# A soft-capped attention and a squared-ReLU feed-forward on one core: another order of the seven products, and sums' transfers on ScalarE's queue

## The chip, the cores and the metric

One core of a Trainium2 chip. The metric is the device time of one launch in microseconds: the median of the runs shown. The profile is one further execution under the hardware profiler; its engines are TensorE (PE; its weight loads PEld), VectorE (DVE), ScalarE (ACT), GpSimd (POOL) and SyncE (SP), which only issues DMAs.

## The reference

For 4 batches, 12 heads, 448 positions and head size 64, everything in fp32:

```
scores = tanh(q k^T / 8 / cap) * cap
attn   = softmax(scores) v                    # per head
x      = heads side by side: 1792 x 768
h      = relu(x w_in)                         # w_in 768 x 2048
g      = s * h^2 + b
y      = g w_out                              # w_out 2048 x 768
```

## The kernel before

**Numbers.** fp32 precision is reached with pairs of fp32r values: every operand of the two big layers is split into a high part (rounded) and a low part (the rest), and a product is three matmuls: hi*hi, lo*hi, hi*lo. ScalarE mostly makes the high parts, DVE the low ones.

**Attention and layer 1.** The 24 pairs of heads are worked off one after another, and beside the attention of a batch TensorE works on layer 1 of the batch before: 16 hidden tiles (128 features x 448 positions), each of 6 x 3 matmuls (L715 to L717), two PSUM banks in turn. ScalarE takes the ReLU out of PSUM (`rectify`, L907) and squares it (L910) into one of three buffers, and SyncE stores it to `hidden_scratch` (`store_hidden`). Behind the last pair of heads the 16 hidden tiles of batch 3 remain: a stretch of TensorE work with little beside it.

**Layer 2** is a fast matrix product of the Strassen-Winograd kind. y is cut in halves of its features (3 accumulators of 128 each), the contraction over 2048 in two halves (8 tiles each), and the positions in batches; a pair of batches (0,1) or (2,3) gives one 2 x 2 problem, solved with seven products instead of eight. A step is one product i (0 to 6) for one pair (0 or 1): 8 tiles of g, each used in 3 x 3 matmuls (L741 to L743, 9 starts). 14 steps are 112 tiles and 1008 matmuls. The order is product by product, each for pair 0 and then pair 1. Tiles are numbered n from 0 to 111 throughout.

The products 3 to 6 need sums of hidden tiles, and 2 to 5 sums of weight tiles. GpSimd makes them in one buffer, `work`: two loads, four adds or subtracts (L1247 to L1253, or L1238 to L1244 for weights), two stores to `t_scratch` or `s_scratch`, and only then the next item. 24 items are listed in `COMBINED`: eight of weights, eight of each pair. SyncE issues their loads (`combine_load`, L388) and stores (`combine_store`, L409); a load waits until the item before has landed in DRAM, a store until GpSimd is done.

**The pipeline of a g tile n.** SyncE loads the raw tile into one of 7 buffers (`load_g`) once ScalarE and DVE are done with tile n-7. ScalarE makes x_hi = s*raw + b (`g_high`, L925; L927 where the product needs no b) in a ring of 6 tiles, once TensorE is done with tile n-6. DVE makes x_lo: for biased products (i < 4) s*raw + b first (L1097), then minus x_hi (L1102); for others one instruction (L1105). Weights come in steps of two tiles: a load (`load_w_out`), w_hi on ScalarE (L915), w_lo on DVE (L1089), 28 steps in all. They go into the place of w_in as its tiles are used up, four products' worth.

**Where products end.** Each step's three accumulators are taken out of PSUM: products 0 and 2 by a copy on ScalarE (`copy_out`), the others by sums on DVE (`add_up`, L1115 to L1139). y is put together in 18 tiles that lie where attention's buffers were (`y_places`), and SyncE stores them (`store_y`). Each pair has three banks of its own; a step waits for the step of its pair before.

**Who does what when** is written out by hand, in each engine's own program. SyncE, in the last stretch of layer 1: three weight steps and g tiles 0 to 6 first; then, for each of 16 hidden tiles, its store, at places a further weight step, and at every fourth a store and a load of a sum. In layer 2 it runs over n: a g load, at places a weight step, a store of y, and every eighth tile a store and a load of a sum, all in one queue. ScalarE and DVE convert four weight steps and g tiles 0 to 5 beside layer 1, the rest in layer 2.

Of the kernel before, what the change touches and what calls it, by code (L numbers as in the profile page):

```python
# [61 lines left out]
STEPS = PRODUCTS * HALVES  # L62
LAST = STEPS * HALF

BIASED = 4 * HALVES * HALF
# [8 lines left out]
COMBINED = ([(-1, k) for k in range(6)] + [(0, k) for k in range(HALF)] + [(-1, k) for k in range(6, HALF)]  # L74
            + [(1, k) for k in range(HALF)])
# [4 lines left out]
def attention_ffn(nc, lead, q_k, v, w_in, w_out, y_t):  # L80
# [5 lines left out]
    with ctx:  # L86
# [56 lines left out]
        y_places += [turned[:], xt[:], r_sum[:, 0, :], r_sum[:, 1, :], e_sum[:, 1, 0, :], e_sum[:, 1, 1, :]]  # L143
        y_places += [hidden_sb[:, u, :] for u in range(3)] + [v_flat[:, u * S:(u + 1) * S] for u in range(2)]
# [64 lines left out]
        p_copied = sem("p_copied")  # L209
# [53 lines left out]

        def hidden_tile(n):
            return hidden_sb[:, n % 3, :]
# [17 lines left out]
        def acc(pair, d):  # L283
            return (scores[:, d, :] if pair == 0 else scores[:, ACCS, :] if d == 0 else pv[:, d - 1, :])[:, 0:S]
# [34 lines left out]
        def free_w_place(eng, m):  # L319

            i, t = divmod(m, W_STEPS)
            if i < W_BUFFERS:
                eng.wait_ge(hid_done, (B - 1) * JT + W_STEPS * i + t + 1)
            else:
                eng.wait_ge(out_used, HALVES * HALF * (i - W_BUFFERS + 1))
# [7 lines left out]
        def w_step_at(n):  # L333

            m, off = divmod(n - RING, W_STEPS)
            m += W_STEPS
            return m if off == 0 and m < W_STEPS * PRODUCTS else None

        def step_at(n):

            step, off = divmod(n - RING + 1, HALF)
            return step - 1 if off == 0 and step > 0 else None

# [3 lines left out]
        def _(sp):  # L347
# [36 lines left out]
            def store_hidden(n):  # L384
                sp.wait_ge(sq_done, n + 1)
                sp.dma_start(hidden[n % JT, :, n // JT * S:(n // JT + 1) * S], hidden_tile(n)).then_inc(hidden_out[n % 3], 16)

            def combine_load(m):  # L388
                pair, k = COMBINED[m]
                if m == 0:  # L390

                    sp.wait_ge(w_in_lo, PIECES)
                else:
                    sp.wait_ge(combine_out, 32 * m)
                if pair >= 0:
                    for batch in (2 * pair, 2 * pair + 1):
                        for j in (k, HALF + k):
                            n = batch * JT + j
                            sp.wait_ge(hidden_out[n % 3], 16 * (n // 3 + 1))
# [582 lines left out]
        def _(dve):  # L982
# [208 lines left out]
            for m in range(W_STEPS):  # L1191
                w_out_low(m)
# [91 lines left out]
```

## Time and profile before

| | us |
|---|---|
| median of 3 runs (lowest, highest) | 599.15 (598.55, 599.56) |
| the profiled execution's own time | 600.41 |
| its span, first to last instruction | 598.6 |
| TensorE with a matmul under way | 587.4 (98%) |
| DVE | 428.2 (72%) |
| ScalarE | 338.3 (57%) |
| GpSimd | 180.1 (30%) |

The profiled execution has 1.8 us outside its span. A share over the whole span hides the stages: the windows below show some of them. Matmuls overlap, so a matmul of some 365 ns starts each 203 ns, and the starts, not the durations, show the pace. The granted clock is 1.00 nearly throughout.

### The profile page before, as it was taken

To read this page: it belongs to the slowest core of one execution; us is meant where nothing else is said; L and a number is where in the kernel's file an instruction comes from. 1 tells how busy PE (TensorE), PEld (TensorE's weight loads), DVE (VectorE), ACT (ScalarE), POOL (GpSimd) and SP (SyncE) were. 2 spreads that over 40 slices of the span, in tenths; PEclk is the share of its full clock that TensorE was granted. 3 is DMA by queue.
4 is the path that set the end of the run, shared out by engine and by line. 5 is a ranking of instruction groups with operands and counts; after the bars stand their busy time and mean duration, and the time that the engine had idled before them with its cause. 6 is when DMAs were issued, how large, how long until landed. Compare 5 with 4: busy or idle time off the path is not lost.

```text
span 598.6 us, 8830 instructions
## 1 busy us (share of the span) xinstructions
PE 587.4 (98%) x3074; PEld 467.9 (78%) x3074; DVE 428.2 (72%) x645; ACT 338.3 (57%) x406; POOL 180.1 (30%) x143
## 2 busy tenths in 40 slices
PE   8999999999999999999999999989999999999997
PEld 4335768677877868868769999979988998999996
DVE  5986999977686869778872033359999889766652
ACT  7985775775575575575652344455545554444430
POOL 0114976303433343434343332333333330000000
PEclk9999999999999999999999999999999999999999
DMA  8432454443545455565445967498898887766532
GB/s 295 154 111 71 120 166 158 133 149 138 191 175 212 163 193 211 208 211 213 165 150 192 350 219 230 178 332 310 306 335 299 279 307 263 225 223 196 173 106 89
DMA packets 63036, 122.71 MB, mean 205 GB/s; under 512 B 6609, under 2 KB 44561, under 8 KB 62993
## 3 DMA queue, kind: packets, MB, share of 16 engines
q1 hardware_dynamic: 62992, 122.16, 59.4%
q8 instruction: 25, 0.41, 0.3%
q14 instruction: 19, 0.15, 0.1%
HBM read 80.97 MB, written 41.16 MB: 204 GB/s over the span
## 4 chain that ended last, share of the span: by engine, by line
PE 61%; DMA 19%; POOL 10%; DVE 3%; ACT 3%; issue 2%; SPq 2%; DVEq 0%; ACTq 0%
PE banks L715 9%; PE banks L717 9%; PE banks L716 9%; DMA work<-hidden_scratch 8%; PE banks L660 8%; DMA t_scratch<-work 7%; PE banks L741 5%; PE banks L743 5%; PE banks L742 5%; PE banks L616 5%; POOL work L1253 2%; POOL work L1249 2%; POOL work L1251 2%; POOL work L1247 2%; DMA work<-w_out 2%
## 5 line engine op out<-in xcount | busy, mean ns | idle before, releaser
L715 PE MATMUL banks<-x_hi,w_hi 128*128 128x448 f32 x384 | 142.6, 371 | 0.0
L717 PE MATMUL banks<-x_hi,w_lo 128*128 128x448 f32 x384 | 140.4, 366 | 0.0
L716 PE MATMUL banks<-x_lo,w_hi 128*128 128x448 f32 x384 | 140.3, 365 | 0.0
L741 PE MATMUL banks<-x_hi,w_hi 128*128 128x448 f32 x336 | 123.7, 368 | 4.8 <-DVE x_lo L1102 4.8
L743 PE MATMUL banks<-x_hi,w_lo 128*128 128x448 f32 x336 | 123.2, 367 | 0.0
L742 PE MATMUL banks<-x_lo,w_hi 128*128 128x448 f32 x336 | 123.2, 367 | 0.0
L907 ACT ACTIVATE hidden_sb<-banks 128x448 f32<-128x448 f32 x64 | 34.8, 544 | 122.0 <-PE banks L717 114.7
L715 PEld LDWEIGHTS banks<-x_hi,w_hi 128*128 128x128 f32 x384 | 72.1, 188 | 20.3 <-issue 14.0
L925 ACT ACTIVATE x_hi<-e,beside 128x448 fp32r<-128x448 f32 x64 | 47.5, 759 | 56.9 <-DMA e<-hidden_scratch 32.6
L901 ACT ACTIVATE e<-e,beside 128x1792 f32<-128x1792 f32 (+1 forms) x48 | 76.2, 1607 | 1.2
L717 PEld LDWEIGHTS banks<-x_hi,w_lo 128*128 128x128 f32 x384 | 72.1, 188 | 6.0
L716 PEld LDWEIGHTS banks<-x_lo,w_hi 128*128 128x128 f32 x384 | 72.1, 188 | 5.5
L741 PEld LDWEIGHTS banks<-x_hi,w_hi 128*128 128x128 f32 x336 | 63.1, 188 | 12.4 <-ACT x_hi L925 3.2
L743 PEld LDWEIGHTS banks<-x_hi,w_lo 128*128 128x128 f32 x336 | 63.1, 188 | 5.7
L742 PEld LDWEIGHTS banks<-x_lo,w_hi 128*128 128x128 f32 x336 | 63.1, 188 | 5.6
L1102 DVE TENSOR_TENSOR x_lo<-e_sum,x_hi 128x448 fp32r<-128x448 f32 x64 | 48.8, 763 | 24.8 <-ACT x_hi L925 17.2
L1247 POOL TENSOR_TENSOR work<-work 128x448 f32<-128x448 f32 x16 | 20.3, 1268 | 150.2 <-DMA work<-hidden_scratch 150.2
L660 PE MATMUL banks<-e,v_sb 128*64 128x448 f32 x288 | 59.4, 547 | 0.3 <-DVE turned L1018 0.3
L927 ACT ACTIVATE x_hi<-e,beside 128x448 fp32r<-128x448 f32 x48 | 32.2, 670 | 47.6 <-PE banks L743 46.1
L1089 DVE TENSOR_TENSOR w_lo<-e,w_hi 128x768 fp32r<-128x768 f32 x28 | 28.8, 1030 | 37.9 <-ACT w_hi L915 37.7
L1097 DVE TENSOR_SCALAR e_sum<-e,beside 128x448 f32<-128x448 f32 x64 | 44.0, 688 | 9.3 <-DMA e<-hidden_scratch 8.0
L1105 DVE SCALAR_TENSOR_TENSOR x_lo<-e,beside,x_hi 128x448 fp32r<-128x448 f32 x48 | 31.7, 682 | 25.3 <-ACT x_hi L927 25.3
(110 smaller groups left out, 787.9 us busy)
## 6 DMA issues: line engine op xcount, KB each, us to landing
hidden_scratch<-hidden_sb SPq DMA_DIRECT2D x64, 224.0 KB, 2.1
work<-hidden_scratch SPq DMA_DIRECT2D x32, 448.0 KB, 4.0
t_scratch<-work SPq DMA_DIRECT2D x32, 448.0 KB, 3.2
e<-t_scratch SPq DMA_DIRECT2D x64, 224.0 KB, 4.1
e<-hidden_scratch SPq DMA_DIRECT2D x48, 224.0 KB, 5.3
beside<-q_k SPq DMA_DIRECT2D x23, 448.0 KB, 4.8
work<-w_out SPq DMA_DIRECT2D x16, 384.0 KB, 3.8
s_scratch<-work SPq DMA_DIRECT2D x16, 384.0 KB, 2.9
```

The lines of the kernel that those rows point to most:

```text
L660: last = nc.tensor.matmul(out[rows], v_sb[:, i, tile:tile + D], e[:, tile_of(p, t, head), :], start=t == 0, stop=False)
L715: nc.tensor.matmul(out, w_hi[:, j, w], x_hi[:, batch % 2, c, :], start=c == 0, stop=False)
L716: nc.tensor.matmul(out, w_hi[:, j, w], x_lo[:, batch % 2, c, :], start=False, stop=False)
L717: last = nc.tensor.matmul(out, w_lo[:, j, w], x_hi[:, batch % 2, c, :], start=False, stop=c == CT - 1)
L741: nc.tensor.matmul(out, w_tile(w_hi_flat, i, k, d), ring(x_hi, n), start=k == 0, stop=False)
L742: nc.tensor.matmul(out, w_tile(w_hi_flat, i, k, d), ring(x_lo, n), start=False, stop=False)
L743: last = nc.tensor.matmul(out, w_tile(w_lo_flat, i, k, d), ring(x_hi, n), start=False, stop=k == HALF - 1)
L901: nc.scalar.activation(e[:, group_of(p, group), :], e[:, group_of(p, group), :], ACT.Exp, scale=cap_c).then_inc(exp_done, 1)
L907: nc.scalar.activation(hidden_tile(n), hid[:, n % 2, 0:S], ACT.Relu).then_inc(relu_done, 1)
L925: nc.scalar.activation(ring(x_hi, n), raw(n), ACT.Identity, scale=s_c, bias=b_c).then_inc(g_hi_done, 1)
L1097: nc.vector.tensor_scalar(g_tile(n), raw(n), s_c, b_c, ALU.mult, ALU.add).then_inc(g_done, 1)
L1102: nc.vector.tensor_tensor(ring(x_lo, n), g_tile(n), ring(x_hi, n).bitcast(F32), ALU.subtract).then_inc(g_lo_done, 1)
```

## The change

1. `ORDER` sets the steps: (0,0) (1,0) (2,0) (0,1) (3,0) (1,1) (4,0) (2,1) (5,0) (3,1) (6,0) (4,1) (5,1) (6,1), product and pair. A g tile is biased by its product, no longer by n < 64.
2. The accumulators of the steps take all eight PSUM banks in turn. A step's bank d waits for what took out the accumulator eight places before.
3. Product 1's sum goes to the place of the second sum, not the third, and product 2's copy, which follows into the same place, waits until that sum has been stored.
4. Twelve weight steps are converted beside the last 16 hidden tiles, one per tile (`W_FIRST`), fifteen are loaded there; the others follow at tiles given by `w_at`. g tiles 7 to 12 are loaded there too.
5. Of batch 3 the first eight hidden tiles are not stored: they stay in eight of the y places (`stays`, `b12_place`), and GpSimd reads them there. DVE waits for GpSimd to be done before it writes over them.
6. `COMBINED` has all weight items first, then pair 0, then pair 1. The store and load of sums, beside layer 1, come at every fifth hidden tile. Behind layer 1 ScalarE issues them, on its own DMA queue: after g_high of tiles 7, 16, 25, ... the store, after 10, 19, 28, ... the load.

```diff
-STEPS = PRODUCTS * HALVES
+ORDER = ((0, 0), (1, 0), (2, 0), (0, 1), (3, 0), (1, 1), (4, 0), (2, 1), (5, 0), (3, 1), (6, 0), (4, 1), (5, 1), (6, 1))
+STEPS = len(ORDER)
...
+W_FIRST = 3
-COMBINED = ([(-1, k) for k in range(6)] + [(0, k) for k in range(HALF)] + [(-1, k) for k in range(6, HALF)]
-            + [(1, k) for k in range(HALF)])
+COMBINED = [(pair, k) for pair in (-1, 0, 1) for k in range(HALF)]
...
+        def stays(n):
+            return (B - 1) * JT <= n < (B - 1) * JT + HALF
+        def b12_place(k):
+            return second_sum(1, k) if k < 2 else third_sum(0, k - 2) if k < 2 + ACCS else third_sum(1, k - 2 - ACCS)
...
-        def acc(pair, d):
-            return (scores[:, d, :] if pair == 0 else scores[:, ACCS, :] if d == 0 else pv[:, d - 1, :])[:, 0:S]
+        def acc(step, d):
+            return banks[:, (step * ACCS + d) % BANKS, 0:S]
...
+        def w_at(m):
+            i, t = divmod(m, W_STEPS)
+            return (RING + W_STEPS if i < W_BUFFERS else HALF * (ORDER.index((i - W_BUFFERS, HALVES - 1)) + 1) + RING
+                    ) + W_STEPS * t
...
@@ SyncE, beside the last 16 hidden tiles
             for j in range(JT):
-                store_hidden((B - 1) * JT + j)
-                if W_STEPS < j <= 2 * W_STEPS:
-                    load_w_out(W_RAW + j - W_STEPS - 1)
-                if j % 4 == 1:
-                    combine_store(combined + j // 4)
-                if j % 4 == 2:
-                    combine_load(combined + j // 4 + 1)
-            combined += JT // 4
-            for n in range(RAW, LAST):
+                if not stays((B - 1) * JT + j):
+                    store_hidden((B - 1) * JT + j)
+                else:
+                    sp.wait_ge(sq_done, (B - 1) * JT + j + 1)
+                if 2 <= j < W_FIRST * W_STEPS + W_RAW - 1:
+                    load_w_out(j + 1)
+                if j >= JT - RING:
+                    load_g(RAW + j - (JT - RING))
+                if j % 5 == 1:
+                    combine_store(sp, combined)
+                    combined += 1
+                if j % 5 == 2:
+                    combine_load(sp, combined)
+            for n in range(RAW + RING, LAST):
                 load_g(n)
...
-                if n % HALF == 6 and combined < len(COMBINED):
-                    combine_store(combined)
-                    combined += 1
-                if n % HALF == 0 and n > HALF and combined < len(COMBINED):
-                    combine_load(combined)
@@ ScalarE
             for j in range(JT):
                 rectify((B - 1) * JT + j)
-                if W_STEPS <= j < 2 * W_STEPS:
-                    w_out_high(j - W_STEPS)
-                if 2 * W_STEPS < j <= 2 * W_STEPS + RING:
-                    g_high(j - 2 * W_STEPS - 1)
+                if 1 <= j <= W_FIRST * W_STEPS:
+                    w_out_high(j - 1)
+                if j > JT - RING - 2 and j < JT - 1:
+                    g_high(j - (JT - RING - 1))
+            combined = COMBINED.index((1, 0))
             for n in range(RING, LAST):
-                if w_step_at(n) is not None:
-                    w_out_high(w_step_at(n))
+                for m in w_steps_at(n):
+                    w_out_high(m)
                 g_high(n)
+                if n % 9 == 7 and combined < len(COMBINED):
+                    combine_store(act, combined)
+                    combined += 1
+                if n % 9 == 1 and combined < len(COMBINED):
+                    combine_load(act, combined)
```

## Rows read from the trace of the kernel before

**Rows 1.** The page's first part: busy us (share of the span) and instructions.
```profile
PE 587.4 (98%) x3074; PEld 467.9 (78%) x3074; DVE 428.2 (72%) x645; ACT 338.3 (57%) x406; POOL 180.1 (30%) x143
```

**Rows 2.** Timeline of TensorE, layer 2: start us, us, instruction [idle before <-releaser].
```profile
382.91 0.36 PE L741 MATMUL banks<-x_hi,w_hi 128*128 128x448 f32 x1
...
395.47 0.36 PE L743 MATMUL banks<-x_hi,w_lo 128*128 128x448 f32 x1
397.76 0.44 PE L741 MATMUL banks<-x_hi,w_hi 128*128 128x448 f32 x1 [1.93 <-DVE x_lo L1102]
...
444.66 0.45 PE L741 MATMUL banks<-x_hi,w_hi 128*128 128x448 f32 x1 [0.80 <-DVE x_lo L1102]
...
457.49 0.37 PE L743 MATMUL banks<-x_hi,w_lo 128*128 128x448 f32 x1
458.48 0.44 PE L741 MATMUL banks<-x_hi,w_hi 128*128 128x448 f32 x1 [0.62 <-DVE x_lo L1102]
...
502.27 0.44 PE L741 MATMUL banks<-x_hi,w_hi 128*128 128x448 f32 x1 [1.46 <-DVE x_lo L1102]
...
502.97 0.37 PE L741 MATMUL banks<-x_hi,w_hi 128*128 128x448 f32 x1
...
595.14 0.37 PE L743 MATMUL banks<-x_hi,w_lo 128*128 128x448 f32 x1
```

**Rows 3.** Windows: from:to, length, busy us by engine, clock, DMA share, GB/s.
```profile
324.00:383.00 59.00, 59.00 (x293) 54.69 (x292) 12.85 (x16) 24.68 (x42) 19.23 (x17) 1.00 0.74 252
...
405.00:465.00 60.00, 58.58 (x287) 53.15 (x286) 55.86 (x78) 31.53 (x46) 20.92 (x16) 1.00 0.92 316
```

**Rows 4.** Timelines of SyncE's queue and of ScalarE, where g tiles came late.
```profile
384.15 1.78 SPq L386 DMA_DIRECT2D hidden_scratch<-hidden_sb  x1
388.55 0.80 SPq L406 DMA_DIRECT2D work<-hidden_scratch  x2
...
389.93 1.88 SPq L455 DMA_DIRECT2D e<-hidden_scratch  x4
...
395.05 2.07 ACT L925 ACTIVATE x_hi<-e,beside 128x448 fp32r<-128x448 f32 x3 [9.29 <-DMA e<-hidden_scratch]
...
491.96 0.80 SPq L416 DMA_DIRECT2D t_scratch<-work  x2
495.69 1.75 SPq L455 DMA_DIRECT2D e<-t_scratch  x4
```

**Rows 5.** Timeline of DVE, without and with GpSimd at work beside it.
```profile
417.14 0.51 DVE L1097 TENSOR_SCALAR e_sum<-e,beside 128x448 f32<-128x448 f32 x1
...
418.32 0.51 DVE L1097 TENSOR_SCALAR e_sum<-e,beside 128x448 f32<-128x448 f32 x1
...
424.77 1.34 DVE L1097 TENSOR_SCALAR e_sum<-e,beside 128x448 f32<-128x448 f32 x1
...
427.53 1.35 DVE L1097 TENSOR_SCALAR e_sum<-e,beside 128x448 f32<-128x448 f32 x1
```

**Rows 6.** Timeline of SyncE's queue: the longest cycle of a sum.
```profile
448.99 0.80 SPq L406 DMA_DIRECT2D work<-hidden_scratch  x2
...
459.37 0.91 SPq L416 DMA_DIRECT2D t_scratch<-work  x2
...
465.94 1.51 SPq L406 DMA_DIRECT2D work<-hidden_scratch  x2
```

**Rows 7.** Groups of instructions by form: count, busy us, mean ns, idle before.
```profile
L1089 DVE TENSOR_TENSOR w_lo<-e,w_hi 128x768 fp32r<-128x768 f32 x28 | 28.8, 1030 | 37.9 <-ACT w_hi L915 37.7
L1105 DVE SCALAR_TENSOR_TENSOR x_lo<-e,beside,x_hi 128x448 fp32r<-128x448 f32 x48 | 31.7, 682 | 25.3 <-ACT x_hi L927 25.3
L1118 DVE TENSOR_TENSOR beside<-beside,banks 128x448 f32<-128x448 f32 x3 | 1.8, 614 | 0.0
L915 ACT CAST w_hi<-e 128x768 fp32r<-128x768 f32 x28 | 23.1, 824 | 0.0
L925 ACT ACTIVATE x_hi<-e,beside 128x448 fp32r<-128x448 f32 x64 | 47.5, 759 | 56.9 <-DMA e<-hidden_scratch 32.6 <-DMA e<-t_scratch 16.3 <-PE banks L743 7.9
```

More of the change, by code:

```diff
@@ L324, in free_w_place, with biased, nth_biased @@
             else:
-                eng.wait_ge(out_used, HALVES * HALF * (i - W_BUFFERS + 1))
+                eng.wait_ge(out_used, HALF * (ORDER.index((i - W_BUFFERS, HALVES - 1)) + 1))
+        def biased(n):
+            return ORDER[n // HALF][0] < BIASED
+        def nth_biased(n):
+            return sum(biased(of) for of in range(n + 1))
         def acc_complete(eng, step, d):
@@ L331, in acc_complete, with w_steps_at @@
                 eng.wait_ge(out_used, (step + 1) * HALF)
[L333 to L337, printed above, removed]
+        def w_at(m):
+            i, t = divmod(m, W_STEPS)
+            return (RING + W_STEPS if i < W_BUFFERS else HALF * (ORDER.index((i - W_BUFFERS, HALVES - 1)) + 1) + RING
+                    ) + W_STEPS * t
+        def w_steps_at(n):
+            return [m for m in range(W_FIRST * W_STEPS, PRODUCTS * W_STEPS) if w_at(m) == n]
         def step_at(n):
@@ L440, in load_g @@
                 step, k = divmod(n, HALF)
-                i, pair = divmod(step, HALVES)
+                i, pair = ORDER[step]
                 reach(sp, g_hi_done, n - RAW + 1)
@@ L457, in store_y @@
             def store_y(step):
-                i, pair = divmod(step, HALVES)
+                i, pair = ORDER[step]
                 for d in range(ACCS):
@@ L750, in out_ready @@
                 n = step * HALF + k
-                m = step // HALVES * W_STEPS + k // W_TILES
-                if step % HALVES == 0 and k % W_TILES == 0:
+                i, pair = ORDER[step]
+                m = i * W_STEPS + k // W_TILES
+                if pair == 0 and k % W_TILES == 0:
                     pe.wait_ge(w_out_hi, m + 1)
@@ L1108, in add_up @@
             def add_up(step):
-                i, pair = divmod(step, HALVES)
+                i, pair = ORDER[step]
                 for d in range(ACCS):
@@ L1189, in _ @@
                     invert(p + 1)
[L1191 to L1194 removed]
+            for j in range(JT):
+                if 1 <= j <= W_FIRST * W_STEPS:
+                    w_out_low(j - 1)
+                if j > JT - RING - 2 and j < JT - 1:
+                    g_low(j - (JT - RING - 1))
             for n in range(RING, LAST):
[L1197 to L1198 removed]
+                for m in w_steps_at(n):
+                    w_out_low(m)
                 g_low(n)
                 step = step_at(n)
[L1201 removed]
+                if step is not None and ORDER[step][0] not in (0, 2):
                     add_up(step)
@@ L1231, in _ @@
                 low(piece)
-            for m, (pair, _) in enumerate(COMBINED):
+            for m, (pair, k) in enumerate(COMBINED):
                 width = HALF_DM if pair < 0 else S
```

195 lines of the change are left out of this document (110 added, 85 removed).

## The prediction
> **What bounds the kernel now.** I read the page's busy shares first [rows 1]: TensorE has a matmul under way for 587.4 of 598.6 us, so an engine beside it can only matter where it makes TensorE wait. The list of waits, cut to TensorE, has one item of size, four waits for DVE's x_lo in the second layer; the timeline of TensorE says where [rows 2], and the four idle times there are 1.93 + 0.80 + 0.62 + 1.46 = 4.8 us. The second layer's 1008 matmuls start between 382.91 and 595.14. The first 62 intervals take 395.47 - 382.91 = 12.56 us, or 202.6 ns each; 1007 such intervals would take 204.0 us, and they take 212.2. So 8.2 us are lost there, and no more can come back in this layer. They have two parts. The starts after a wait (tile 7 at 397.76, tile 32 at 444.66, tile 39 at 458.48, tile 62 at 502.27), with small slips around them, hold 6.1 us (the first alone, 397.76 - 395.47, is 2.29 where 0.20 is due). The rest is a slower pitch: from 502.97 to the end 446 intervals take 92.17 us, 206.7 ns each. It began with the wait before 502.27 and stayed. It also shows between the waits at 444.66 and 458.48: 62 intervals to 457.49 take 12.83 us, 206.9 ns. (206.7 - 202.6) ns x (448 + 62) is 2.1 us. Both pitches are at a granted clock of 1.00, the 2.4 GHz level, so it isn't the clock gate; I take it that a wait can leave TensorE in either pitch.
>
> Why DVE is late differs by place. At tile 7 it is SyncE's order [rows 4]: behind the store of a hidden tile at 384.15, SyncE waits until 388.55 for a sum's store to land before it can load the next sum, by its program has the last hidden tile's store next, and only at 389.93 begins the g loads from tile 7 on; ScalarE gets tile 7 at 395.05, after 9.29 us of waiting. At tile 62 the same: a store of sums at 491.96, the next g loads only at 495.69. At tiles 32 and 39 it is DVE itself: busy 55.9 of 60 us between 405 and 465 [rows 3]. A biased tile costs it 1.18 us from start to start, and 2.76 us while GpSimd works on a sum [rows 5]. So for a product of 8 tiles (14.6 us of TensorE) it needs 8 x 1.18 = 9.4, plus two tiles at 1.58 more for a sum = 3.2, plus two w_lo at 1.03 = 2.1 [rows 7]: 14.7 us, and 1.8 more wherever product 1's three sums of 0.61 us follow. It can't refill the lead it never had after tile 7.
>
> **The change part by part.** Matmuls, their count and order in layer 1, and the end of the kernel stay; 3.5 us from the last matmul's start to the span's end (598.6 - 595.14) are kept.
>
> *First g tiles.* SyncE now issues the loads of tiles 7 to 12 in the loop over the last 16 hidden tiles, one per 3.65 us hidden tile. The gap at tile 7 goes, 2.09 us, and with it the slips right behind it and at tile 8, 0.28 by the same intervals: 2.4 us. What is late next is tile 13, whose load waits for DVE's tile 6, some 3 us after layer 2 begins; it lands 5 to 6 us later, and ScalarE wants it when tile 7 is used up, at 8 x 1.82 = 14.6 us. Covered.
>
> *Twelve weight steps converted beside layer 1, where there were four.* That puts 8 x 1.03 on DVE and 8 x 0.82 on ScalarE into a stretch of 59 us in which they are busy 12.9 and 24.7 [rows 3, 7]. Per hidden tile of 3.65 us ScalarE had 24.7 / 16 = 1.5; with a weight step (0.82) and a g tile (0.76) on top of that it is 3.1 at most. SyncE may come late with a weight step while it waits at a sum; two PSUM banks let ScalarE be 3 us late. I take nothing; the upper bound is one such lateness, 2 us. It takes 8.2 us off DVE in layer 2.
>
> *Batch 3's first eight hidden tiles stay in SBUF.* Eight stores and eight half loads of 224 KB go, and for those tiles ScalarE waits for no store. GpSimd's work is unchanged. No TensorE wait hangs on it: 0.
>
> *The interleaved order of products and eight banks in turn.* DVE's demand by product, with a sum each 9 tiles (2.8 us per 8): (1,0) 14.3; (2,0) 16.1 with product 1's three sums; (0,1) 12.2; (3,0) 13.2; (1,1) 18.0 with product 3's six sums (3.7) and two weight steps; (4,0), unbiased at 0.68 a tile, 12.1; (2,1) 18.0 with product 4's six; (5,0) 10.3; (3,1) 15.2. Against 14.6 the arrears are at most 1.5 in the first part, 3.4 at (1,1) and 3.4 - 2.5 + 3.4 = 4.3 at (2,1). The lead: a tile may be made once the tile six before it is used, so it has 5 x 1.82 = 9.1 us less 0.76 and 0.63 for itself, 7.7 us. 4.3 is under 7.7, so tiles 32 and 39 lose their stalls, if the lead is whole at the start. A bank comes free two and two thirds products later instead of two: no wait. ScalarE's copy of product 2 waits for the store of product 1's sum to have landed, 8 tiles after that sum, 14.6 us for a 3 to 4 us store: none.
>
> *Sums issued by ScalarE.* Eight sums (one stored, seven loaded and stored) now stand in ScalarE's queue: the store at tiles 7, 16, ..., the load at tiles 10, 19, .... Two pairs of DMA issues at 0.80 us a pair [rows 6] are 1.6 us per 16.4 us, in an engine with 31.5 busy of 60 [rows 3]; hidden. Each adds waits, and what is queued behind is x_hi, then DVE's x_lo, then TensorE. From load to store there are 6 tiles, 10.9 us; the longest cycle before needed 459.37 - 448.99 = 10.4. From store to load 3 tiles, 5.5 us; it needed 465.94 - 459.37 = 6.6 [rows 6]. So about 1 us of waiting in the worst cycle, out of a lead of 7.7: 0. Bounds: for a cycle C it is 7 x (C - 16.4) - 7.7 if positive, which is 0 for the longest cycle in the rows, 17.0, and 14 us for one of 19.5, as far above as the mixture of two queues might make it; I take the end that the rows are at, 0. The other side is SyncE: it no longer stops, so tile 62's wait goes, 1.7 us with the slip behind it. The last sum is stored near tile 64 of TensorE; its first reader in (3,1) is wanted from tile 73 on, 16 us later.
>
> The Trainium skill, page "DMA: Bandwidth & Descriptors", section "Issuing engines are not separate DMA queues", holds that issuing from several engines saves only the issuing time, since all use the same DMA engines. By that alone, this part is worth four issues of 0.40 us per sum on SyncE, where nothing waits for them: nothing. The gain above is of another kind, waits in order, so it stands if transfers are not what is late; case (b) below is the one in which they are.
>
> **Sum.** -2.4 (tile 7) - 1.1 - 1.0 (tiles 32, 39 with slips) - 1.7 (tile 62) - 2.1 (pitch) is -8.3 with rounding; the difference of the starts, 212.2 - 204.0 = 8.2, is the exact one. Span 590.4; the profiled execution 600.4 - 8.2 = 592.2. The three unprofiled runs have a median of 599.15, 1.26 below the profiled one, so the same step gives **591.0 us**, 589.8 to 592.5 on its own: a slower pitch in layer 1's stretches can come or go for under 1 us, and one small slip may stay.
>
> **Rivals.** (a) *A stall is left and brings the slower pitch.* The DVE burst near (1,1), where six sums, two weight steps and a sum on GpSimd fall together, is the likeliest place. 1 us, and 4.1 ns x about 590 matmuls = 2.4: 594.5. For it: of the four waits two, at 444.66 and 502.27, left the slow pitch behind them. Against: arrears of 4.3 us in a lead of 7.7.
> (b) *Transfers stay late.* DMA engines are busy 0.92 of the time from 405 to 465 [rows 3]; ScalarE waited 32.6 us in all for g loads from hidden_scratch [rows 7], and its own queue now competes with them. Then DVE's lead is not whole, and tiles 32 and 39 or their successors stall and leave the slow pitch: only 2.4 + 1.7 come back: 595 to 596. Against: 3.1 MB of weight loads and 3.6 MB of hidden tiles leave that stretch.
> (c) *Slower: ScalarE stands in the sums' cycle.* Loads, GpSimd, stores take longer than 16.4 us in the new mixture, every cycle holds x_hi up, and TensorE starves. Loss 7 x (C - 16.4) - 7.7; it passes 8.2 from C = 18.7 us on. At C = 19.5 the time is 599.15 - 8.2 + 14.0 = 605. The longest cycle in the rows is 17.0 [rows 6].
> (d) *The sums aren't ready for (3,1)*, so the interleaving doesn't do what it says: a wait of some 6 us at tile 72 and the slow pitch for 40 tiles, 4.1 ns x 360 = 1.5: 591.0 + 7.5 = 598.5, no change.
>
> **How the numbers follow.** Forecast 0.62, (a) 0.17, (b) 0.10, (c) 0.06, (d) 0.05. Under 0.2% (1.2 us) can't be told from no change here. Faster: 0.62 + 0.17 + 0.09 + 0.01, rounded to 0.88; same 0.05; slower 0.07. The range 589.8 to 595.5 holds the forecast, (a) and half of (b).
>
> **What would show it.** Right: no TensorE wait over 0.5 us after layer 1, tile 1007's start some 204 us after the first, pitch 202.6 ns throughout; ScalarE waits for a sum's store at most about 1 us at a time; SyncE has no wait of 3 us and more before a g load that is due; DVE busy near tile 48 without a gap on TensorE. Wrong: ScalarE idle for GpSimd or for a store of sums by 3 us a cycle (c); ScalarE waiting for g loads as long as before, 32.6 us in all (b); a wait at tile 72 to 79 for a load from the sums (d); a stall in the last 16 hidden tiles behind a weight step.

## The result, and the profile after

Over 14 runs of each kernel, on the same chips, the changed kernel takes a median of **595.83 us** (594.04 to 597.84) and the one before 599.34 (597.79 to 602.81): a ratio of 0.9938, 95% interval 0.992 to 0.9956. It is faster, as forecast, but by 3.5 us where 8.2 were forecast, and 595.83 lies above the forecast range of 589.8 to 595.5.

The profiled execution of the changed kernel took 595.86 us, with a span of 594.1. The page's first part, which answers to [rows 1]:

```profile
PE 585.0 (98%) x3074; PEld 468.5 (79%) x3074; DVE 424.6 (71%) x645; ACT 339.7 (57%) x406; POOL 182.4 (31%) x143
```

It is nearly the same page, since the same work is done. The timeline of TensorE in the second layer shows more. These rows answer to [rows 2]; the layer's matmuls now stand on lines 787 to 789:

```profile
383.70 0.36 PE L787 MATMUL banks<-x_hi,w_hi 128*128 128x448 f32 x1
...
467.40 0.37 PE L789 MATMUL banks<-x_hi,w_lo 128*128 128x448 f32 x1
469.40 0.44 PE L787 MATMUL banks<-x_hi,w_hi 128*128 128x448 f32 x1 [1.64 <-DVE x_lo L1161]
...
471.13 0.37 PE L789 MATMUL banks<-x_hi,w_lo 128*128 128x448 f32 x1
472.16 0.44 PE L787 MATMUL banks<-x_hi,w_hi 128*128 128x448 f32 x1 [0.66 <-DVE x_lo L1161]
...
590.59 0.37 PE L789 MATMUL banks<-x_hi,w_lo 128*128 128x448 f32 x1
```

The layer takes 590.59 - 383.70 = 206.9 us where it took 212.2, and 1007 intervals of 202.7 ns would be 204.1. The four waits before are gone, and so is the slower pitch. Two new waits stand in their place, at tiles 46 and 47, the last two of product (1,1): from start to start 2.00 and 1.03 us where 0.20 is due, and 2.8 us with the slips next to them. They are all that is lost in this layer. The layer also begins 0.8 us later than before (383.70 against 382.91); that shift is there from the first matmuls of the hidden layer on (50.39 against 49.60) and stays the same through layer 1, so it comes from what lies ahead of them, when the kernel's first loads landed. It is no effect of the change: in a second execution of the kernel before the hidden layer starts at 50.52, and 49.60 is the earliest of all executions here.

The windows that answer to [rows 3], with the same columns:

```profile
324.00:383.00 59.00, 59.00 (x293) 54.69 (x292) 20.32 (x25) 30.83 (x50) 18.60 (x14) 1.00 0.82 280
405.00:465.00 60.00, 60.00 (x298) 55.62 (x297) 49.51 (x74) 30.11 (x45) 17.03 (x13) 1.00 0.77 259
```

DVE and ScalarE are busier in the last 59 us of layer 1 (20.3 and 30.8 against 12.9 and 24.7), and no stall came of it. Behind it DVE is down from 55.9 to 49.5 of 60 us, and the DMA share from 0.92 to 0.77. ScalarE's waits for a g load fell from 32.6 + 16.3 us to these, from the list of waits (us in all, times, longest):

```profile
ACT x_hi L975 <- DMA e<-t_scratch: 1.4, 1, 1.4
ACT x_hi L973 <- DMA e<-hidden_scratch: 1.0, 1, 1.0
```

In their place the same list has five groups which the kernel before could not have, because ScalarE now issues the sums' transfers. L1320 is GpSimd's last addition of a sum, and `t_scratch<-work` is a sum's store:

```profile
ACT x_hi L973 <- POOL work L1320: 7.4, 3, 2.6
...
ACT w_hi L963 <- POOL work L1320: 2.5, 1, 2.5
ACT x_hi L975 <- DMA t_scratch<-work: 2.5, 1, 2.5
...
ACT hidden_sb L983 <- DMA t_scratch<-work: 1.4, 1, 1.4
...
ACT x_hi L975 <- POOL work L1320: 1.4, 1, 1.4
```

That is 15.2 us in which ScalarE, with the x_hi behind, stood still for a sum. How one such wait reaches TensorE some 27 us later is seen in three timelines of the changed kernel. First ScalarE, its queue of DMA issues among its work:

```profile
429.31 0.46 ACTq L397 DMA_DIRECT2D work<-hidden_scratch  x1
...
441.86 0.81 ACTq L407 DMA_DIRECT2D t_scratch<-work  x2
442.78 2.07 ACT L973 ACTIVATE x_hi<-e,beside 128x448 fp32r<-128x448 f32 x3 [5.16 <-PE banks L789]
445.41 0.35 ACTq L394 DMA_DIRECT2D work<-hidden_scratch  x1
...
446.30 1.41 ACT L983 COPY hidden_sb<-banks 128x448 f32<-128x448 f32 x3 [1.45 <-DMA t_scratch<-work]
```

Then GpSimd, the four additions of the same sum:

```profile
436.33 1.47 POOL L1314 TENSOR_TENSOR work<-xt,work 128x448 f32<-128x448 f32 x1 [13.28 <-DMA work<-hidden_scratch]
...
440.63 1.20 POOL L1320 TENSOR_TENSOR work<-work 128x448 f32<-128x448 f32 x1
```

The load issued at 429.31 had landed when GpSimd began at 436.33, 7.0 us later. The last addition ends at 440.63 + 1.20 = 441.83, and at 441.86 ScalarE issues the store, with x_hi right behind. The idle time of 5.16 us before that x_hi is put down to TensorE's bank, but the store ahead of it shows what ended it: GpSimd. The list of waits therefore understates the sums: this x_hi comes 4.1 us later against TensorE than one that waited for nothing. Then DVE:

```profile
443.57 0.63 DVE L1161 TENSOR_TENSOR x_lo<-e_sum,x_hi 128x448 fp32r<-128x448 f32 x1 [2.76 <-ACT x_hi L973]
...
448.46 0.96 DVE L1148 TENSOR_TENSOR w_lo<-e,w_hi 128x768 fp32r<-128x768 f32 x1 [1.90 <-ACT w_hi L963]
...
462.83 0.61 DVE L1180 TENSOR_TENSOR beside<-beside,banks 128x448 f32<-128x448 f32 x1
...
466.41 0.95 DVE L1148 TENSOR_TENSOR w_lo<-e,w_hi 128x768 fp32r<-128x768 f32 x1
467.28 0.51 DVE L1156 TENSOR_SCALAR e_sum<-e,beside 128x448 f32<-128x448 f32 x1
467.92 1.34 DVE L1161 TENSOR_TENSOR x_lo<-e_sum,x_hi 128x448 fp32r<-128x448 f32 x1
```

Call lead the time from the end of a tile's x_lo to the start of TensorE's first matmul of that tile. A whole lead is 7.4 us (tile 13, for one). It falls from 6.2 us at tile 34 to 3.3 at tile 35, the x_lo of 443.57 above, and to 2.4 at tile 38, after the w_lo that waited 1.90 us. Two tiles beside GpSimd's work then take it to 0.5 at tile 40, with nothing to spare and no wait, and at tile 45 it has grown back to 2.9. Then come the six sums of product 3 and a w_lo (462.83 to 467.28, 4.45 us), and GpSimd's next sum slows tile 46's x_lo to 1.34 us. Tile 46 is ready 6.3 us after tile 45, where TensorE takes 1.8: 4.5 us of arrears at once, against a lead of 2.9.

### The profile page after: what moved, and what is told of

It reads as the page before. It is cut to its first block, busy times and chain, and to the rows that moved or that the text cites. A ratio compares the mean times of both kernels' runs of the same rounds, so it can differ in the third digit from the quotient of the medians.

```text
span 594.1 us, 8822 instructions
## 1 busy us (share of the span) xinstructions
PE 585.0 (98%) x3074; PEld 468.5 (79%) x3074; DVE 424.6 (71%) x645; ACT 339.7 (57%) x406; POOL 182.4 (31%) x143
## 4 chain that ended last, share of the span: by engine, by line
PE 91%; DVE 4%; ACT 2%; issue 1%; DMA 1%; SPq 0%; DVEq 0%; ACTq 0%
PE banks L749 14%; PE banks L751 13%; PE banks L750 13%; PE banks L787 11%; PE banks L788 11%; PE banks L789 11%; PE banks L694 8%; PE banks L650 5%; PE banks L716 2%; PE banks L674 1%; DMA work<-w_in 1%; PE banks L596 1%; DVE e_sum L1060 1%; ACT e L948 1%; ACT e L925 1%
## 5 line engine op out<-in xcount | busy, mean ns | idle before, releaser
L749 PEld LDWEIGHTS banks<-x_hi,w_hi 128*128 128x128 f32 x384 | 72.1, 188 | 20.3 <-issue 14.0
L955 ACT ACTIVATE hidden_sb<-banks 128x448 f32<-128x448 f32 x56 | 30.5, 544 | 98.7 <-PE banks L751 98.7
L1164 DVE SCALAR_TENSOR_TENSOR x_lo<-e,beside,x_hi 128x448 fp32r<-128x448 f32 x48 | 33.1, 708 | 24.3 <-ACT x_hi L975 24.3
L694 PEld LDWEIGHTS banks<-e,v_sb 128*64 128x64 f32 x288 | 18.7, 136 | 32.3 <-issue 32.3
```

Of the source, the lines that this page charges most:

```text
L694: last = nc.tensor.matmul(out[rows], v_sb[:, i, tile:tile + D], e[:, tile_of(p, t, head), :], start=t == 0, stop=False)
L749: nc.tensor.matmul(out, w_hi[:, j, w], x_hi[:, batch % 2, c, :], start=c == 0, stop=False)
L1164: nc.vector.scalar_tensor_tensor(ring(x_lo, n), raw(n), s_c, ring(x_hi, n).bitcast(F32), ALU.mult, ALU.subtract).then_inc(g_lo_done, 1)
```

## The experiments

The rows above hold two candidates for the missing 2.8 us: ScalarE's waits, which had used up the lead, and the burst itself. A third is chance, since one profile shows one execution. The first four kernels were made to tell these apart, and the early g loads from the rest of the change.

**The changed kernel again**, with no edit.

> The changed kernel once more, as the mark for the others on this chip. Expected near its median of 595.8 us, 3.5 below the kernel before. Theory 1 and theory 2 (see the two kernels beside it) both expect TensorE to stall at tiles 46 and 47 again, about 1.8 and 0.8 us, since what leads there (six sums of product 3, a weight step and GpSimd's work on DVE) is in the program and not in chance. If the stalls are elsewhere or absent in this execution, their place is chance, and single profiles may not be compared by them.

Measured: 596.93 us (594.07 to 600.86, 12 runs), ratio 0.9964 (0.9942 to 0.9986). The profiled execution (596.09) stalls at tiles 46 (2.2 us with slips) and 47 (0.9) and nowhere else, so the stalls belong to the kernel and not to one execution.

**SyncE issues the sums**, at the same tiles by ScalarE's count, everything else as changed. The block in ScalarE's program goes; SyncE's loop over g tiles gets it:

```diff
             for n in range(RAW + RING, LAST):
                 load_g(n)
+                if (n - RAW) % 9 == 7 and combined < len(COMBINED):
+                    combine_store(sp, combined)
+                    combined += 1
+                if (n - RAW) % 9 == 1 and n > RAW + 1 and combined < len(COMBINED):
+                    combine_load(sp, combined)
...
-                if n % 9 == 7 and combined < len(COMBINED):
-                    combine_store(act, combined)
-                    combined += 1
-                if n % 9 == 1 and combined < len(COMBINED):
-                    combine_load(act, combined)
```

> Undoes one part: the stores and loads of sums behind layer 1 are issued by SyncE again, at the same tiles by ScalarE's count (SyncE is seven tiles ahead, so at tiles 14, 23, ... and 17, 26, ...). All else as changed. Theory 1: ScalarE standing in its queue for GpSimd and for the store of sums (some 4 us near tile 34 to 37, 1.5 to 2.9 elsewhere) used up DVE's lead before the burst at tile 45; then the stalls at tiles 46 and 47 go or halve, ScalarE shows no wait for GpSimd, and the time is 1.5 to 2.8 us below the changed kernel, about 593.5. Theory 2: the burst of six sums with a weight step and GpSimd beside it is enough by itself; then the stalls stay and the time is that of the changed kernel within 0.7 us. Rival of both: SyncE stops at sums again and g loads come late as in the kernel before; then ScalarE waits for DMAs and the time is above the changed kernel by 1 to 3 us.

Measured: **593.03 us** (592.71 to 593.25, 6 runs), ratio 0.9904 (0.9886 to 0.9922), 593.05 in the profiled execution. That is 2.8 us below the changed kernel's profiled execution and 3.9 below its median measured beside it (596.93). Its TensorE, first matmul of the layer, the stretch where tile 47 begins, and the last one:

```profile
383.72 0.36 PE L792 MATMUL banks<-x_hi,w_hi 128*128 128x448 f32 x1
...
469.24 0.36 PE L794 MATMUL banks<-x_hi,w_lo 128*128 128x448 f32 x1
469.44 0.36 PE L792 MATMUL banks<-x_hi,w_hi 128*128 128x448 f32 x1
...
587.80 0.36 PE L794 MATMUL banks<-x_hi,w_lo 128*128 128x448 f32 x1
```

204.08 us, without a stall, at 202.7 ns. Its window answers to the second one above:

```profile
405.00:465.00 60.00, 60.00 (x298) 55.60 (x297) 53.04 (x78) 31.09 (x45) 18.12 (x14) 1.00 0.78 263
```

DVE got 3.5 us more done by the same moment, with ScalarE hardly busier: before, it had waited. Lead at tile 45 is 5.8 us; the same burst takes it to 2.0 at tile 46, still above nothing. SyncE bears the sums' waits easily, as its queue shows:

```profile
446.12 0.32 SPq L394 DMA_DIRECT2D work<-hidden_scratch  x1
...
458.11 0.90 SPq L407 DMA_DIRECT2D t_scratch<-work  x2
...
466.22 0.32 SPq L394 DMA_DIRECT2D work<-hidden_scratch  x1
```

A cycle of 20.1 us from load to load here is longer than any on ScalarE (16.1 to 18.3), yet x_hi isn't late: SyncE's g loads are issued tiles ahead of ScalarE's need.

**DVE's sums at a step's end spread over three tiles**, one accumulator behind each, for every step that has them. ScalarE's issues are left in place: this takes away the burst, the other candidate.

```diff
-                step = step_at(n)
-                if step is not None and ORDER[step][0] not in (0, 2):
-                    add_up(step)
+                for d in range(ACCS):
+                    step = step_at(n - d)
+                    if step is not None and ORDER[step][0] not in (0, 2):
+                        add_up(step, [d])
```

> The changed kernel, but DVE takes a finished step's three accumulators out one per tile (behind tiles 8s+13, +14, +15) instead of all three behind the first. That moves 2.4 us of DVE work behind tile 46 and 1.2 us behind tile 47. Theory 2 (the burst): both stalls go, about 593.0 us. Theory 1 (the lead was used up before): the stall at tile 46 shrinks from 1.8 us to nothing too, but ScalarE's waits stay and the rest of the arrears appears one or two tiles later, so 0.5 to 1 us of stall is left: about 594.

Measured: 593.16 us (592.27 to 594.71, 6 runs), ratio 0.9907 (0.9887 to 0.9927); layer 2 takes 204.09 us without a stall. ScalarE still waits for the sums, and the lead is 4.7 us at tile 45 and 1.2 at its lowest, at tile 50. So neither cause makes the stall alone. It takes both, and removing either brings all of it back.

**The kernel before with the early g loads alone.**

```diff
+                if j >= JT - RING:
+                    load_g(RAW + j - (JT - RING))
...
-            for n in range(RAW, LAST):
+            for n in range(RAW + RING, LAST):
```

> One part alone in the kernel before: SyncE issues the g loads of tiles 7 to 12 in the loop over the last 16 hidden tiles. The order of steps, banks, weight steps and sums stay as before. By the prediction's step this takes away the stall at tiles 7 and 8, 2.4 us, and with DVE's lead whole the arrears to tile 39 (0.1 us per product, 1.8 for each set of three sums) stay under 7.7 us, so tiles 32 and 39 don't stall either and only tile 62 (SyncE's order) is left with the slow pitch behind it: 4.4 us below the kernel before, 594.9. Rival: DVE can't keep TensorE's pace in that stretch in any case, the stalls only move later, and 2 us or less come back: 597.3.

Measured: 598.06 us (596.56 to 600.68, 12 runs), ratio 0.9993 (0.9975 to 1.0012): no difference. The expectation was missed by 3 us. Tile 7's stall is gone, and there is one ahead of it, in layer 1. TensorE's timeline of that kernel, then ScalarE's:

```profile
344.86 0.47 PE L717 MATMUL banks<-x_hi,w_hi 128*128 128x448 f32 x1 [0.52 <-ACT hidden_sb L909]
```

```profile
344.26 0.54 ACT L909 ACTIVATE hidden_sb<-banks 128x448 f32<-128x448 f32 x1 [6.03 <-DMA hidden_scratch<-hidden_sb]
```

ScalarE waits 6.03 us for the store of a hidden tile before it can write the next one, and TensorE then lacks a bank. The edit can't be the cause of this stall, which comes 27 us before the first of the early loads, here in SyncE's queue:

```profile
372.41 0.75 SPq L455 DMA_DIRECT2D e<-hidden_scratch  x1
```

The kernel before has the same wait on ScalarE, only shorter:

```profile
341.95 0.55 ACT L907 ACTIVATE hidden_sb<-banks 128x448 f32<-128x448 f32 x1 [5.12 <-DMA hidden_scratch<-hidden_sb]
```

TensorE begins a hidden tile every 3.65 us, the sixth of the last 16 at 342.78 by counting back from 382.91, and ScalarE had freed the bank at 341.95 + 0.55 = 342.50. So by this estimate the kernel before escaped the stall by 0.3 us in that execution. Stalls at tiles 38, 39 and 62 (0.5 to 1.1 us) stay, as does a pitch of 206.7 ns over the 197 intervals between tiles 40 and 62.

**The kernel before once more**, one execution.

> The kernel before once more, one profile. The prediction took 1.26 us off because the profiled execution of the kernel before (600.41) lay above the median of its runs, and took its layer 2 to begin at 382.91. Theory A: single executions of this kernel differ by where it stalls and where the slow pitch follows, and by when the first loads land; then this profile has stalls at tiles 7, 32 to 40 and 62 again but other stretches at 206.7 ns, its layer 2 begins 0.5 to 1.4 us later than 382.91 (as in four other executions, 383.5 to 385.1), and its time is 597 to 600 us. Theory B: the profile adds a fixed 1.3 us to every execution; then it has the same stretches and about 600.4 us. (The kernel with sums on SyncE speaks against B already: profiled 593.06, median 593.03.)

Measured: 596.99 us, against 600.41 in the execution shown of before. Its layer 2 takes 207.9 us, not 212.2, with waits at tiles 7, 31, 40 and 62, of which none is over 0.9 us; tiles 7 and 62 lose 0.2 us each, where the forecast took 2.1 and 1.7 for them. The 4.4 us less in layer 2 and 1.0 of later start make up the whole 3.4 between the two executions. ScalarE's wait for a hidden tile's store is there again (4.89 us), without a stall. Neither execution is the typical one: 600.41 lies 1.1 above the median of 14 runs, and 596.99 lies 3.0 below that of the 17 runs beside it (599.98).

**The kernel before with early g loads and twelve weight steps beside layer 1**, all sums of weights first in the list of sums, the order of products unchanged. A part of the edit:

```diff
+W_FIRST = 3
...
-                if W_STEPS <= j < 2 * W_STEPS:
-                    w_out_high(j - W_STEPS)
+                if 1 <= j <= W_FIRST * W_STEPS:
+                    w_out_high(j - 1)
```

> Two parts of the change in the kernel before: g loads of tiles 7 to 12 and the conversion of twelve weight steps (instead of four) beside the last 16 hidden tiles, with all weight sums ahead in the list of sums. The order of steps stays product by product, sums on SyncE every eighth tile. If DVE's load in the first 60 tiles is what empties its lead (8.2 us of w_lo are moved out of layer 2), tiles 32 to 40 don't stall, and only tile 62, where the last sums are due, stalls with the slow pitch behind it or not: 2.5 to 5 us below the kernel before, 594 to 597. If the order of steps is what relieves DVE, stalls at tiles 38 to 40 stay as in the kernel with early g loads alone (1.6 us there) and the time is about 598.

Measured: 598.93 us (597.83 to 601.36, 12 runs), ratio 0.9991 (0.9971 to 1.0011). Layer 2 has no stall, and yet takes 593.54 - 385.43 = 208.11 us, because every one of its 1007 intervals is 206.7 ns long. Layer 1 has two stalls in which TensorE waits for a bank. Ahead of the first ScalarE had waited 4.61 us for a hidden tile's store, ahead of the second 4.14 us for the load of a weight step (its w_hi at 368.46):

```profile
343.95 0.47 PE L717 MATMUL banks<-x_hi,w_hi 128*128 128x448 f32 x1 [0.49 <-ACT hidden_sb L909]
370.44 0.48 PE L717 MATMUL banks<-x_hi,w_hi 128*128 128x448 f32 x1 [0.55 <-ACT hidden_sb L909]
```

The slow pitch begins behind the second. Two waits of half a microsecond thus come with a loss of some 6 us: 2.1 between the first matmul of layer 1 and that of layer 2 (335.4 against 333.3 in the changed kernel), and 4.0 in layer 2.

**Sums on ScalarE's queue, a cycle of ten tiles instead of nine.** If the queue itself is what's slow, this changes nothing in a load's landing; if the cycle is too tight, it is enough.

```diff
-                if n % 9 == 7 and combined < len(COMBINED):
+                if n % 10 == 7 and combined < len(COMBINED):
...
-                if n % 9 == 1 and combined < len(COMBINED):
+                if n % 10 == 0 and combined < len(COMBINED):
```

> The changed kernel, sums still issued by ScalarE, but a store and a load every ten tiles instead of nine: load at tiles 10, 20, 30, ..., store at 17, 27, 37, .... From load to store there are now 7 tiles, 12.8 us, instead of 10.9. Theory 1 (ScalarE's wait for GpSimd empties the lead before tile 45): x_hi stays within 1.5 us of its full lead, the x_lo lead before tile 45 is 4.5 us or more instead of 2.9, no stall at tiles 46 and 47, time about 593.2 with a narrow spread like the kernel with sums on SyncE. Rival (the place of the queue itself, contention of two queues for the DMA engines, is the cost): loads of sums on ScalarE's queue still land in 5.7 us and the stalls stay: 595 to 596. A risk of its own: the last sum is stored at tile 77 and first read for tile 79; if that comes late there is a stall at tile 79.

Measured: 593.22 us (593.02 to 593.65, 6 runs), ratio 0.9896 (0.9868 to 0.9925); layer 2 takes 204.08 us without a stall, and the lead is 5.6 us at tile 45. One tile more between load and store, 1.8 us, is enough. ScalarE's remaining waits for a sum, from the list:

```profile
ACT w_hi L963 <- POOL work L1320: 2.6, 1, 2.6
ACT x_hi L975 <- POOL work L1320: 2.5, 1, 2.5
ACT x_hi L973 <- DMA t_scratch<-work: 2.3, 1, 2.3
```

**SyncE's sums and the spread together.**

> Both edits that each took the stalls away: sums issued by SyncE and the take-out of a step's accumulators spread over three tiles. Each alone gives layer 2 in 204.1 us, which is the pace of the matmuls, so nothing is left to gain: 593.0 us within 0.4, with the smallest lead in layer 2 above 2 us instead of 1.6 and 1.2. If it is slower, stores of y that come later hold SyncE up.

Measured: 593.28 us (592.59 to 593.58, 6 runs), ratio 0.9894 (0.9868 to 0.992). The lowest lead rises to 3.5 us, and nothing is gained by it: where no wait is left, more lead is worth nothing.

**The sums on SyncE, but no tiles kept in SBUF.** This undoes the step that the forecast set at 0: all 64 hidden tiles go through DRAM again.

> The kernel with sums on SyncE (593.0 us), with one more part undone: all 16 last hidden tiles are stored to DRAM again, and GpSimd's loads for pair 1 are whole again. The prediction set this part at 0. In e4 and e6, which store all 16 and load g early, ScalarE waited 4.6 to 6.0 us for a hidden tile's store, TensorE stalled in the last 16 hidden tiles by 0.5 to 0.7 us once or twice, and a slow pitch followed. Theory: the same here, since SyncE's queue is the same in that stretch: one or two stalls of 0.5 to 0.7 us before layer 2, and the slow pitch in whole or in part behind it: 593.7 to 598.5 us. Rival (the prediction's 0): no stall before layer 2, 593.0 to 593.4.

Measured: 594.51 us (593.56 to 599.07, 7 runs), ratio 0.9922 (0.9905 to 0.9939), 1.5 us above the same kernel with the tiles kept; its lowest run is above the other's highest. The two were measured on different chips, and the intervals of their ratios overlap, so the size is uncertain: by the ratios it is 1.1 us. The profiled execution is its slowest, 599.07, and shows what the kept tiles are good for:

```profile
344.88 0.47 PE L754 MATMUL banks<-x_hi,w_hi 128*128 128x448 f32 x1 [0.51 <-ACT hidden_sb L960]
```

It is the wait of the kernels above, at the same place; here too ScalarE had waited 5.00 us for the store of a hidden tile. Of the six profiled executions that store all 16 last hidden tiles, those of the kernel before included, all have such a wait on ScalarE (4.6 to 6.0 us) and four a stall of TensorE behind it; of the eight in which the first eight stay, none has either. Layer 2 has no stall and takes 208.1 us, all at 206.7 ns.

**What brings the slow pitch.** Three kernels give TensorE extra waits. The first two are the kernel with SyncE's sums, plus ten waits for the x_lo of the tile five ahead, at the first matmul of every tenth tile, or inside it:

```diff
+PULSES = ((10, 0), (20, 0), (30, 0), (40, 0), (50, 0), (60, 0), (70, 0), (80, 0), (90, 0), (100, 0))
...
+                if (n, d) in PULSES:
+                    pe.wait_ge(g_lo_done, n + RING)
```

> The kernel with sums on SyncE (layer 2 without a stall, 204.1 us, pitch 202.7 ns) with ten deliberate waits of TensorE: at the start of tiles 10, 20, ..., 100 it waits until DVE is done with the tile five ahead, which takes about 1.5 us of idle each while DVE and ScalarE make that tile. It measures the slow pitch by itself. Theory A (a wait can leave TensorE in either pitch until its next wait): some of the ten stretches between waits run at 202.6 and some at 206.7 ns, none between. Layer 2 then takes 204.1 + 10 x 1.7 = 221 us plus 0.37 us for every slow stretch of 90 matmuls. Theory B (the slow pitch comes from what other engines do in those stretches, as between tiles 39 and 62): all stretches run at 202.6, or slow ones begin and end inside a stretch.

> As the kernel with ten deliberate waits, but the waits stand inside the tiles: before the second or the third group of three matmuls of tiles 10, 20, ..., 100 in turn, so that they are shorter, about 1.0 and 0.4 us. Other lengths of wait, same question: if the pitch behind a wait is drawn anew each time, the slow stretches fall at other tiles than in that kernel; if it depends on the tile (what the other engines do there), at the same ones.

> The kernel before with early g loads and twelve early weight steps (e6: 597.0 us of span, all 1007 intervals of layer 2 at 206.7 ns and no stall) with one deliberate wait of TensorE, at the start of tile 1 of layer 2, until DVE is done with tile 6: about 1.6 us. Theory A (a wait draws the pitch anew): if it lands on the fast pitch, the 1.7 us wait gives back up to 4.1 us, so the time is up to 2.4 us below e6, 596.5 against 598.9; if it lands on the slow one, it is 1.7 us above e6. In either case all of layer 2 behind the wait has one pitch. Theory B (the other engines' work makes that layer slow): 1.7 us above e6 at 206.7 ns.

The third has one such wait, at tile 1, in the kernel before with early g loads and weights. Measured: 631.06 and 617.00 us in one execution each; 600.59 for the third (597.89 to 603.92, 12 runs), ratio 1.0033 (1.0015 to 1.0051). The waits were longer than meant, up to 5.7 us (from start to start, less the 0.20 due; so with all lengths of these waits below). Behind those at tiles 10, 20 and 40 of the first kernel the pitch was 206.7 ns, behind the seven others 202.6; in the second kernel it was slow behind 10, 20 and 80 and fast behind 40. So a wait can change the pitch, and either level may follow it. Tiles 40 and 80 differ between the two kernels, so the tile alone doesn't set it; tiles 10 and 20 are slow in both. The third shows one change clearly, the last matmul at the fast pitch, the wait, and the last of the layer:

```profile
387.86 0.37 PE L747 MATMUL banks<-x_hi,w_lo 128*128 128x448 f32 x1
389.88 0.44 PE L745 MATMUL banks<-x_hi,w_hi 128*128 128x448 f32 x1 [1.66 <-DVE x_lo L1106]
...
596.21 0.37 PE L747 MATMUL banks<-x_hi,w_lo 128*128 128x448 f32 x1
```

The 998 intervals from 389.88 to 596.21 are 206.7 ns each, where the same kernel had 202.7 ahead of the wait. Its stall in layer 1 at 371.54, at the place of the one that the slow pitch followed in the kernel without the extra wait, had left the fast one.

## Why the prediction was wrong

The profiled execution's 595.86 us less the 591.0 forecast is 4.9 us, and three things make it up: 2.8 of stalls at tiles 46 and 47, 0.8 of a later start, and 1.26 that should not have been taken off.

- **First g tiles, -2.4; tiles 32 and 39, -1.1 and -1.0; tile 62, -1.7; pitch, -2.1.** None of these losses is left in the changed kernel, and the one with the sums on SyncE takes 204.08 us for the layer where the forecast said 204.0. But the sizes were those of one execution (tiles 7 and 62 lose 0.2 us each in the other), and they don't add up part by part. The first g tiles alone bring nothing measurable (0.9993): stalls at tiles 38, 39 and 62 and the slow pitch stay. With the weights it is nothing either (0.9991): two stalls in layer 1 and the slow pitch behind them stand in their place.
- **Twelve weight steps beside layer 1, 0.** Right for the changed kernel, which has no stall there. With all 16 hidden tiles stored, a weight step that came 4.14 us late stalled TensorE by 0.55.
- **Tiles kept in SBUF, 0.** Mis-sized, by 1.1 to 1.5 us. "No TensorE wait hangs on it" was true of the one execution that was read, and by 0.3 us only: ScalarE's wait of 5.12 us for a hidden tile's store was there, and the forecast didn't ask how far it was from stalling TensorE. With the tiles stored four of six profiled executions stall there by some 0.5 us, with eight of them kept none of eight.
- **The interleaved order, arrears of 3.4 us at (1,1).** Mis-sized. They were averaged over a product of eight tiles. The burst behind tile 45 (six sums, a w_lo, and a tile beside GpSimd) takes 3.8 us of lead in one tile with SyncE's sums (5.8 to 2.0) and 4.5 in the changed kernel. Alone it would still have been covered.
- **Sums issued by ScalarE, "about 1 us of waiting in the worst cycle, out of a lead of 7.7: 0".** This is the step that failed. x_hi came some 4.1 us late at tile 35 and again at tile 38: its lead is 4.0 and 3.9 us there, where a whole one is 8.1. The step took the longest cycle of the kernel before as the worst case, split at the two places where ScalarE now waits; the real cycle has its own worst parts (7.0 us for a load to land, 5.5 us for four additions, against 10.9 for both). And it set each wait against a whole lead, though DVE, which needs most of its time here, gives lead back slowly, so that waits and DVE's own arrears add up. Moving the same issues to SyncE, or adding one tile to the cycle, gives back all 2.8 us of the profiled execution. What the changed kernel's slower executions (up to 600.86) lose beyond that no trace shows.
- **Where it would go wrong.** Rival (a), at 0.17, named the place, "the DVE burst near (1,1)", and a stall; it expected 1 us and the slower pitch, and the runs show 2.8 and, in the profiled executions, no slower pitch. Its cause lay half in rival (c), the sums' cycle in ScalarE's queue, which was priced only as a cycle that never fits. Rival (b)'s time of 595 to 596 is the one that was measured, but its mechanism is refuted: the waits for g loads are 2.4 us in all. Rival (d) is refuted too, since TensorE has no wait in product (3,1).
- **From the profiled execution to the median, -1.26.** The difference between one execution and the median of three was carried over as if it belonged to the measurement. It belonged to that execution: its stalls and slow pitch were among the terms that the forecast took away already. In kernels without stalls the profiled execution is like the others (593.05 against a median of 593.03). Without it the forecast is 592.2, and the best kernels are at 593.0 to 593.3 with 0.8 us of later start.

The Trainium skill, page "DMA: Bandwidth & Descriptors", section "Issuing engines are not separate DMA queues", says that all engines' transfers share the same 16 DMA engines, so that issuing from another saves only issue time. The runs agree in the time: with the sums on ScalarE's queue at a cycle of ten tiles, or on SyncE's, it is the same (593.22 and 593.03). What decided here was not the transfers but the order: at 441.86 ScalarE's issue of a store had waited for GpSimd, and the x_hi behind it came 4.1 us late.

**The best version** is the change with the sums on SyncE, 593.03 us, 1% below the kernel before, and 2.8 us below the changed one's first median (595.83), 3.9 below its second (596.93, the one measured beside it). The spread sums, the cycle of ten tiles and the two together are within 0.25 us of it and can't be told from it. All four also spread little: 592.27 to 594.71 over 24 runs, where the kernel before ranges over 5.0 us in the first comparison and the changed kernel over 3.8, and 6.8 in its second.

## What to carry to other kernels

Before a wait is moved into an engine that feeds the critical one, follow the lead tile by tile, with every wait and burst subtracted from what the one before it has left, not from a whole lead; an average over a stage hides the tile in which it runs out. Give waits to the engine whose work is due latest: the same sums cost nothing on SyncE, though a cycle took up to 20.1 us there, and 2.8 us on ScalarE. Ask of a wait that costs nothing how far it is from costing something: here it was 0.3 us. Take a forecast's difference from layers or stages, and don't carry a single execution's distance from the median over to a kernel in which its causes are gone.

## What was not expected of the hardware

- **Two pitches at one clock.** Matmuls of 128x448 follow each other at 202.6 or 206.7 ns, both at a granted clock of 1.00, the 2.4 GHz level. The forecast had this as an assumption from two stretches; seven kernels show it. A change mostly came with a wait, 0.5 us being enough, but in the kernel without kept tiles the pitch went from fast to slow near 356 us, 11 us behind the wait at 344.88 and without a gap. A whole layer of 1007 intervals at the slow pitch costs 4.1 us, more than most waits in it. What sets the level stays open: ten waits in a row left three slow, at tiles 10, 20 and 40 in one kernel and 10, 20 and 80 in the other.
- **After some waits the clock itself fell.** Behind the waits of 5.7 and 4.7 us at tiles 10 and 20 of the kernel with ten waits TensorE ran at half clock. The window behind the first, and a stretch ahead of it:

```profile
396.00:402.00 6.00, 6.00 (x31) 5.57 (x30) 3.06 (x6) 3.92 (x7) 0.89 (x1) 1.00 0.91 288
408.50:412.40 3.90, 3.90 (x12) 3.47 (x11) 0.00 (x0) 0.68 (x1) 0.00 (x0) 0.50 0.24 61
```

0.50 is the 1.2 GHz level, and 12 matmuls in 3.90 us stand against 31 in 6.00. The two waits of 2.3 and 2.2 us at tiles 30 and 50 were followed by it too, 1.2 and 1.5 us after the matmuls had begun again, and those of 5.0 and 3.4 us at tiles 10 and 20 of the kernel with the waits inside tiles, while those of 3.3 us at tile 40, 3.9 at tile 60 and 1.8 later on of the first kernel were not. So the length of the wait alone doesn't decide it.
- **The sums' loads of 448 KB took a little longer on ScalarE's queue.** In layer 2 their median from issue to landing is 5.7 us in the changed kernel, by the list of DMA issues (count, KB each, median us) between 385 and 600 us:

```profile
work<-hidden_scratch ACTq DMA_DIRECT2D x7, 448.0 KB, 5.7
```

The same stretch of the kernel with the sums on SyncE has:

```profile
work<-hidden_scratch SPq DMA_DIRECT2D x7, 448.0 KB, 5.0
```

In the four profiled executions with ScalarE's queue the median is 5.7 to 6.6, in the two with SyncE's and the same loads 5.0 and 4.7. Why is not shown. At a cycle of ten tiles it cost no time (6.2 us there); in the changed kernel the 7.0 us of one load are part of the 12.5 that didn't fit into 10.9.
